# The four-column mask on ScalarE, two first steps of round 2 later on VectorE, a weight piece's low part between g and its low part, and the waits of the merged slots ahead of three wide products on TensorE

## What is computed

```
for t in range(S):
    cur = einsum('bhd,bhe->bhde', u * k[t], v[t])
    y[t] = einsum('bhd,bhde->bhe', r[t], state + cur)
    state = w[t][..., None] * state + einsum('bhd,bhe->bhde', k[t], v[t])
x = y laid out as (3072 tokens, 384)
x = ((x @ w_a) * (x @ w_b)) @ w_out                  # 384 -> 1536 -> 384
h = x @ w_in
out = (maximum(h, 0) + alpha * minimum(h, 0)) @ w_out2   # 384 -> 2048 -> 384
```

## Time and profile before

| | us |
|---|---|
| median of 3 runs | 1011.1 (1010.41 to 1011.45) |
| the profiled execution | 1010.97 |
| its span, first to last instruction | 1009.2 |
| TensorE busy in it | 987.4 (98%) |
| VectorE busy | 586.3 (58%) |
| ScalarE busy | 296.8 (29%) |
| GpSimd busy | 24.1 (2%) |

### The profile page before, as it was taken

How to read it: one execution, slowest core, us unless ns; L and a number is a source line. 1 busy time by engine, 2 the same in 40 slices (tenths; PEclk the granted TensorE clock), 3 DMA queues, 4 the chain that set the end, 5 groups by cost and what they waited for, 6 DMA issues and landing times.

```text
span 1009.2 us, 26702 instructions
## 1 busy us (share of the span) xinstructions
PE 987.4 (98%) x11200; PEld 963.8 (96%) x11200; DVE 586.3 (58%) x1209; ACT 296.8 (29%) x628; POOL 24.1 (2%) x24
## 2 busy tenths in 40 slices
PE   5799999999999999999999999999999999999998
PEld 5799999999999999999999999999999999999998
DVE  7796765855857658567432437555555555555554
ACT  3435314223242242341223324222222222222212
POOL 4400000000000000000000000000000000000000
PEclk9999999999999999999999999999999999999999
DMA  6554311312113013110020414010101010101000
GB/s 174 144 149 121 93 38 34 111 30 65 53 29 92 25 36 87 53 37 2 25 60 15 128 32 126 8 40 11 38 13 35 13 34 14 32 16 32 20 6 23
DMA packets 42126, 52.88 MB, mean 52 GB/s; under 512 B 5152, under 2 KB 42016, under 8 KB 42016
## 3 DMA queue, kind: packets, MB, share of 16 engines
q1 hardware_dynamic: 40624, 51.04, 17.7%
q10 hardware_dynamic: 1392, 0.25, 0.2%
HBM read 39.48 MB, written 9.44 MB: 48 GB/s over the span
## 4 chain that ended last, share of the span: by engine, by line
PE 95%; DVE 3%; issue 1%; ACT 0%; ACTq 0%; DMA 0%; DVEq 0%; SPq 0%
PE products L170 18%; PE products L172 16%; PE products L171 16%; PE acc L170 12%; PE acc L171 12%; PE acc L172 12%; PE products L740 3%; PE products L758 1%; PE products L800 1%; PE products L816 1%; PE products L715 1%; PE products L785 1%; PE products L772 1%; DVE f_y L986 1%; DVE k_in L998 1%
## 5 line engine op out<-in xcount | busy, mean ns | idle before, releaser
L170 PE MATMUL products<-x_parts,weights_hi 128*128 128x384 f32 x576 | 202.2, 351 | 2.6 <-DMA x_parts<-f_y 2.0
L172 PE MATMUL products<-x_parts,weights_lo 128*128 128x384 f32 x576 | 195.1, 339 | 0.3 <-issue 0.3
L171 PE MATMUL products<-x_parts,weights_hi 128*128 128x384 f32 x576 | 194.7, 338 | 0.0
L1375 DVE TENSOR_SCALAR leaky_low<-products,leaky_al 128x384 f32<-128x384 f32 x128 | 79.1, 618 | 169.9 <-PE products L172 169.8
L1322 ACT ACTIVATE leaky_g_hi<-leaky_g_sb 128x384 fp32r<-128x384 f32 x128 | 67.3, 526 | 295.5 <-DVE leaky_g_sb L1380 183.8
L1235 DVE TENSOR_TENSOR g_sb<-a_g,products 128x384 f32<-128x384 f32 x96 | 53.1, 553 | 158.9 <-issue 90.8
L549 ACT ACTIVATE g_hi<-g_sb 128x384 fp32r<-128x384 f32 x96 | 50.3, 524 | 254.5 <-DVE g_sb L1235 254.5
L170 PEld LDWEIGHTS products<-x_parts,weights_hi 128*128 128x128 f32 x576 | 108.0, 187 | 7.8 <-issue 2.7
L172 PEld LDWEIGHTS products<-x_parts,weights_lo 128*128 128x128 f32 x576 | 108.2, 188 | 0.7 <-issue 0.7
L171 PEld LDWEIGHTS products<-x_parts,weights_hi 128*128 128x128 f32 x576 | 108.2, 188 | 0.0
L170 PE MATMUL acc<-g_hi,weights_hi 128*128 128x384 f32 x288 | 96.6, 336 | 0.0
(11 more groups left out here) (94 smaller groups left out, 1757.4 us busy)
## 6 DMA issues: line engine op xcount, KB each, us to landing
k_in<-in_k_dram SPq DMA_DIRECT2D x16, 336.0 KB, 3.9
r_in<-in_r_dram SPq DMA_DIRECT2D x16, 336.0 KB, 5.2
stage<-in_w_out_dram SPq DMA_DIRECT2D x14, 384.0 KB, 3.3
w_v<-in_v_dram SPq DMA_DIRECT2D x16, 288.0 KB, 3.6
y_dram<-x_in SPq DMA_DIRECT2D x8, 576.0 KB, 4.6
x_in<-y_dram SPq DMA_DIRECT2D x8, 576.0 KB, 4.6
out_dram<-leaky_out_sb SPq DMA_DIRECT2D x7, 576.0 KB, 3.3
stage<-in_w_dram SPq DMA_DIRECT2D x10, 336.0 KB, 3.8
```

What stands on the lines that cost most here:

```text
L170: pe.matmul(out, w_hi, x_hi, start=first, stop=False)
L171: pe.matmul(out, w_hi, x_lo, start=False, stop=False)
L172: return pe.matmul(out, w_lo, x_hi, start=False, stop=last)
L1375: dve.tensor_scalar(self.low[f % 2][:, :], h, 0.0, self.al[:, f:f + 1], ALU.min, ALU.mult).then_inc(self.low_ready, 1)
```

## The change

Four edits:

1. `copy_four_mask` goes from VectorE (round 0, phase 7) to ScalarE, behind `prepare_r(0, 1)` at the start.
2. In round 2, `step_r(2, 1, 0)` goes from phase 0 behind `prepare_fours(2, 0)` in phase 1, and `first_step_k(2, 1)` from phase 0 between `merge_fours(2, 0)` and `prepare_fours(2, 1)` in phase 2.
3. The low part of weight piece 6 goes from behind VectorE's work for block 1 to between `g_sb` and `g_lo` of block 2.
4. The five waits at the head of `four` (`wait_four`) are put in `up_b(g)`, ahead of its last three matmuls (`kt == KT - 1`).

```diff
+PUT_OFF = 6
@@ ScalarE
                 prepare_r(0, 1)
                 act.dma_start(ident[:, :], constants[0:ROWS, 0:ROWS]).then_inc(ident_loaded, 16)
+                copy_four_mask()
@@ TensorE
-                def four(n, j, g):
+                def wait_four(n, j):
 
                     pe.wait_ge(merged, merges(n, 0, 3))
                     pe.wait_ge(fours_merged, fours(n, j))
                     pe.wait_ge(k_first[j], n + 1)
                     pe.wait_ge(fours_copied[j], fours_round(n))
                     pe.wait_ge(fours_stepped[j], 2 * fours_round(n))
+
+                def four(n, j, g):
+
                     for c in range(CH):
@@ up_b
                             for block in range(KT):
                                 wait_x(tile + 1, block)
+                        if kt == KT - 1 and step_at(g) is not None:
+                            n, phase = divmod(step_at(g), PHASES)
+                            if n >= FOURS_FROM and phase in (2, 3):
+                                wait_four(n, phase - 2)
                         product = up_part(g, "w_b", b_ps(g), kt)
@@ VectorE, phases 0 to 2
                         if n == 2:
-                            first_steps(n)
+                            first_steps(n, 0)
...
                         if n >= FOURS_FROM:
                             prepare_fours(n, 0)
+                        if n == 2:
+                            step_r(n, 1, 0)
                     elif phase == 2 and n >= FOURS_FROM:
                         merge_fours(n, 0)
+                        if n == 2:
+                            first_step_k(n, 1)
                         prepare_fours(n, 1)
...
-                    elif phase == 7 and n == 0:
-                        copy_four_mask()
@@ VectorE, each block
                         attend_early(step)
+                    if g == 2:
+                        shared.split_lo(dve, PUT_OFF)
                     dve.wait_ge(g_hi_ready, g + 1)
```

More of the change, by code:

```diff
@@ L575, in prepare_r, with copy_four_mask @@
                     scaled(r_leaf[j], queries_of(n, j), 0, j).then_inc(r_prepared[j], 1)
+                def copy_four_mask():
+                    act.wait_ge(masks_loaded, 32)
+                    dims = [2 * FOUR, Q // (2 * FOUR)]
+                    copy(view(four_mask, 0, [dims, [FOUR, 2], [1, FOUR]], P),
+                         view(level_mask, 0, [dims, [0, 2], [1, FOUR]], P)).then_inc(four_mask_ready, 1)
                 def copy_fours(n, j):
@@ L1021, in merge_level @@
                                         view(products, level_bank(phase, 0), [[BANK, 2], [32, 2 * CH], [h, 32 // h], [1, h]], P)).then_inc(merged, 2)
[L1023 to L1028, removed]
                 def prepare_fours(n, j):
@@ L1127, in step_r, with first_steps @@
                     dve.tensor_tensor(halves(t, h, 1), halves(t, h, 1), decay(n, j, h, 0), ALU.mult).then_inc(r_stepped[j], 1)
[L1129 to L1133, removed]
+                def first_steps(n, j):
+                    first_step_k(n, j)
+                    step_r(n, j, 0)
                 def lower_outputs(n):
@@ L1163, in attend @@
                         if n == 1:
-                            first_steps(n)
+                            first_steps(n, 0)
+                            first_steps(n, 1)
                         products_of_w(n, 0, 2 if n < FOURS_FROM else 1, range(1, 7))
@@ L1190, in attend @@
                         copy_last_level(n)
-                    elif phase == 7 and n == 0:
-                        copy_four_mask()
-                    elif phase == 7:
+                    elif phase == 7 and n > 0:
                         step_r(n, 0, 5)
@@ L1245, in _ @@
                         for piece in new_pieces(f):
-                            shared.split_lo(dve, piece)
+                            if piece != PUT_OFF:
+                                shared.split_lo(dve, piece)
                     if tile == TILES - 1 and f < AHEAD:
```

## The result

| us | before | after |
|---|---|---|
| median | 1011.1 (1010.41 to 1012.33, 5 runs) | 1027.37 (1025.97 to 1030.21, 5 runs) |
| profiled execution | 1010.97 | 1030.21 |
| its span | 1009.2 | 1028.4 |
| TensorE busy in it | 987.4 | 994.6 |

After over before is 1.0162, with a 95% interval of 1.0144 to 1.018: 16.3 us more, where I had forecast 10.2, and above my range.

A forecast was written before the change was run, and what follows sets the result against it. TensorE was taken as the bound, busy 987.4 of 1009.2 us. Terms +11.2 + 1.6 - 2.0 - 0.5 = +10.3 us on the profiled 1010.97 gave 1021.3 us, range 1018.5 to 1024.5.

The forecast's parts named there:

- the one on the clock: TensorE behind the new stalls: a clock fall was treated only as a rival, with no term in the sum.
- edit 1: Start, mask copy off VectorE: outputs and their DMAs come sooner, -2.0 us, between 0 and -3.5.
- edit 3: Block 2, near 60 us: TensorE's wait for `g_sb` goes, -0.5 us, between -0.6 and 0.
- The stalls of rounds 3 to 7: Phase 2 of five rounds: TensorE waits for `prepare_fours` with twelve wide matmuls still to do, 11.2 us more.
- Round 2: Moved steps and waits together: the old 0.67 us wait goes, a 2.25 us stall comes, +1.6 us.
- Phase 3: Waits moved three matmuls ahead: the preparation for stream 1 has 0.9 us to spare, so 0 us.
- Rival 2: Clock falls in each of six stalls, 1.65 us lost each: +9.9, so 1031.2 us; 7 in 100.
- the 0.4 us to spare: Round 2, phase 3: margin left after a step is put ahead of `prepare_fours(2, 1)`; no wait, 0 us.
- the range's end of 0: Start: the mask move gains nothing if the DMAs land later, behind the weight piece.
- The fall at 35.5 us: Start: clock at 0.50 from 35.5 to 38.8 us; it may stay at 1.00 with 1.8 us less standstill.
- rival 4: The start brings nothing or costs: +12.3, so 1023.3 us; 15 in 100.

The follow-up runs named there:

- e1: Kernel before with only the waits of `four` moved ahead of the last three matmuls of `up_b`, rounds 2 to 7: 1030.88 us, 1.0196.
- e4: Kernel before with only round 2's two state steps moved, as in the change: 1010.77 us, 0.9996.
- e8: Kernel before with only the phase 3 waits of `four` moved ahead of the last three matmuls of `up_b`: 1011.31 us, 0.9999.
- e2: Kernel after with the waits of `four` put back at the slot's head, the other three edits kept: 1010.6 us, 0.999.
- e9: Kernel before with only the low part of weight piece 6 moved to block 2, mask still on VectorE: 1011.29 us, 0.9998.
- e3: Kernel before with only the mask copy moved from VectorE to ScalarE: 1010.86 us, 0.9994.
- e6: Kernel before with only the phase 2 waits of `four` moved, ahead of the nine matmuls of `down`: 1023.63 us, 1.0118.

## Why the prediction missed

The step that failed is the one on the clock: the sum has no term for a fall behind the stalls, and the runs show some 4.3 us of them. Two terms were mis-sized beside it, edit 1 (-2.0 us, about -0.6 in its place) and edit 3 (-0.5, about 0). The three come to 6.2 us; the median lies 6.1 above the forecast.

**The stalls of rounds 3 to 7: right.** 5 x 2.24 us were forecast; the rounds without a fall measured 2.22 to 2.27, in after and in e1. `four` waits for nothing, the preparation moves along with TensorE, and the row in the view of waits has its six times 2.1 us.

**Round 2: right.** +1.6 forecast. Measured 3.13 with a fall, less 1.5 to 1.6 for it, leaves 1.6. I said that VectorE would idle some 0.3 us ahead of `g_sb`; it was 0.24:

```profile
118.62 0.55 DVE L1246 TENSOR_TENSOR g_sb<-a_g,products 128x384 f32<-128x384 f32 x1 [0.24 <-PE products L173]
```

**Phase 3: right.** 0 forecast and found, in after (no such wait), in e4 (the 0.4 us to spare held) and in e8.

**The clock: the step that failed.** Rival 2 had the mechanism and the price (1.65 us forecast for a fall, 1.5 to 1.6 measured), but I made it one case with six falls or none and gave it 7 in 100, while neither the sum nor the range had a term for a single one. The two rows on which I judged it, 3.2 us idle with a fall and 1.9 us without, bracket 2.25; nothing in them says that all six must come out alike, and one execution's row says little of 1.9 us, as e4 and e2 show. What the runs show is a share of the stalls: 6 of 12 at 2.1 to 2.2 us. Each stall should have carried some half of 1.6 us, 4.8 us for the six. The reason that I gave for less, that wide products stand close on both sides, was in no row, and these six fell in spite of it. The three profiled falls gave 4.6 us, and the mean clocks of the five runs about 2.8 falls, 4.3 us. That the profiled 1030.2 lies near rival 2's 1031.2 is luck: it had three falls and a slow start, not six falls.

**Edit 1: the mechanism right in one profile, the term mis-sized.** I took -2.0 us from a copy of 4.61 us, as though it took that always; it takes 1.04 in about half of the profiles. And I followed the gain to the issue of the DMAs only. Of their landing I had said that it could take back everything (the range's end of 0), and so it did in the profiled execution: 0.07 us were left. The fall at 35.5 us was gone, as I had thought it might be (e9, with the mask on VectorE, hasn't it either), but one of 6.8 us stood behind the longer idle time ahead of the first wide product, where before the clock had stayed at 1.00. This last cost, +2.3 us, was in no bound of mine. In the mean of ten runs edit 1 is -0.6 us, with an interval of -1.6 to +0.3 (e3). On this term rival 4 was nearer than the forecast.

**Edit 3: the wait went, the time did not.** -0.5 forecast, -0.60 found at that place in after, and +0.62 at the next block, where `a_g` stands behind a high part whose piece is late. I had asked what VectorE does with the time and what piece 9 needs, not which engine is next late. ScalarE's wait for the next stage was in the trace of before, 0.74 us at 62.76; without the wait for `g_sb` it was 1.61 in after and 1.54 in e9. e9 has -0.61 and +0.53, and a ratio of 0.9998.

**The sum mended.** 12.8 for the stalls, 4.3 for the falls, -0.6 for edit 1 and 0 for edit 3 are +16.5, against 16.3 measured. The count of falls in runs without a profile rests on a mean clock with three digits and edit 1's term on an interval of 1 us to either side, so an agreement this close is partly luck. The same sum for e1, 13.5 for its stalls (round 2's by 2.2) and 2.9 falls, 4.5, gives +18.0, where 19.4 was measured. What stays open is how the 3.5 us between e1 and after are made up beyond edit 2's 0.7, and what decides in one stall of 2.1 us whether the clock falls: the six stalls of after have the same idle time to 0.01 us (2.07 or 2.08) and came out three and three. Their place in time is the rival that no run tests.

## What to carry to other kernels

A wait may be moved ahead of other work only as far as its condition is already met there; if it isn't, each matmul that stood between is paid in full, in every round. Price an idle stretch of TensorE as its length plus the chance of a fall of the clock, taken from many stalls of that length and not from one, and make it a part of the forecast for each stall, not a rival for all. And before a small stall is booked as a gain, look for the next condition at that place in the trace, and for whether the delay that it rests on is there in more than one execution.

## What the hardware showed that was not expected

- The same 128x32 mask copy on VectorE took 1.03 to 1.04 us in four profiles and 4.60 to 4.61 us in five, at the same place in the order; a GpSimd multiplication 3.5 us earlier told the two apart in all nine (1.23 or 1.24 against 0.85 us).
- Equal stalls don't give equal clocks: 2.07 us idle led to 3.4 us at half clock in three of six cases. A stretch at half clock behind a stall was 3.4 us long every time and cost 1.5 to 1.6 us. At the start of the wide products, 3.32 us of idle time went with one of 6.8 us in after and 3.37 us with one of 3.4 us in e6.
- Moving five semaphore waits from one place to another, where their conditions are met, changed the time by nothing that can be measured (e8, 0.9999, 0.9987 to 1.0011).
